# Gated attention and two expert layers on one core: the experts' first product by a Strassen scheme, seven block products for eight

## The chip, the cores and the metric

The kernel runs on one core of a Trainium2 chip. The metric is the device time of one execution in microseconds; of the kernel before there are three timed runs and one profiled execution.

## What is computed

A gated linear attention, then a bilinear layer, then a layer of four experts. The part that the change touches is the last (x is the output of the bilinear layer, 3072 tokens of 384):

```python
def _moe2_ref(x, domain_probs, w1, w2) -> np.ndarray:
    N, D = x.shape
    E = w1.shape[0]
    p = domain_probs / (domain_probs.sum(-1, keepdims=True) + 1e-09)
    out = np.zeros((N, D), dtype=np.float32)
    for e in range(E):
        h = np.maximum(x @ w1[e], 0.0)
        out += p[:, e:e + 1] * (h @ w2[e])
    return out.astype(np.float32)
```

There are 4 experts, w1[e] is 384 x 1024, w2[e] is 1024 x 384.

## The kernel before

The kernel issues each engine's instructions by hand, in program order, with semaphores between engines. Everything is held transposed: features lie on the 128 partitions, tokens along the columns.

Every product is made of split values: a number is its rounded part (`hi`) plus a rest (`lo`), and a block product is three matmuls, hi by hi, hi by lo, lo by hi (`TERMS`). The hi parts come from ScalarE copies, the lo parts from a difference on VectorE or GpSimd.

*The stage before.* Attention and bilinear layer run together over 4 batches of 768 tokens. A step of the bilinear layer (`up1`, `down1`, `bilinear`) is 27 matmuls of 384 columns: 18 for the two products a and b into banks 0 and 1, and 9 into banks 2 to 4. ScalarE copies a, VectorE multiplies (L838), ScalarE rounds (L607), GpSimd takes the difference g_lo (L528). Each half batch ends with x1, whose hi and lo parts are stored to DRAM by the sync engine (SP). In the last half batch ScalarE and GpSimd also split the first expert's weights (`pieces_high` L578, `pieces_low` L517), 1024 columns a step.

*The experts' stage.* The loops are: expert, pair of token tiles ("round", 512 tokens each tile), tile, and column block f of the 8 blocks of 128 in the 1024. A step (`step2`) is one tile and one f: 9 up matmuls (L1221, three input blocks of 128 by three terms) into bank 0 or 1 by turns, for the step after next, and 9 down matmuls (L1339) into three banks that gather over the 8 f. In `step2` a down matmul and an up matmul follow each other one by one. When a bank is full, VectorE applies relu and gate (L1036), ScalarE rounds to h_hi (L731), VectorE takes h_lo (L1040). For expert 0, ScalarE reads the bank itself (L617) and the gate comes in the sum. After 8 f VectorE adds three banks to `total` in SBUF (L1026, L1028). x1 is loaded from DRAM again for each expert, 24 times hi and lo; the weights of the next expert are loaded in one piece while the present one runs.

At the border of the stages the first up product is issued ahead of the last `down1` (in `bilinear`, where `last_batch and beside and s == STEPS1 - 1`), the second behind it.

## Time and profile before

| | |
|---|---|
| three timed runs, median | 1203.96 us (1203.85 to 1204.05) |
| the profiled execution | 1203.85 us |
| its span, first to last instruction | 1202.1 us |
| granted TensorE clock, mean | 1.000 |
| busy: TensorE / VectorE / ScalarE / GpSimd | 1196.4 / 549.1 / 287.1 / 161.2 us |
| experts' stage | from 413.3 us to the end |

The span is what lies between the first and the last instruction; the execution takes 1.75 us more. "PE" is TensorE's matmuls, "PEld" its weight loads, which run beside the matmuls; DVE is VectorE, ACT ScalarE, POOL GpSimd, and a name with q is that engine's sequencer. A matmul's own duration in the trace reaches past the start of the next, so their pace is read from the starts.

### The profile page before, as it was taken

The page shows a single profiled execution, that of the slowest core. Times are in us where ns is not written, and L with a number is a line of the kernel's source. Part 1 is how long each engine was busy: PE and PEld are TensorE (multiplying, and loading weights), DVE is VectorE, ACT ScalarE, POOL GpSimd, SP SyncE. Part 2 cuts the span into 40 slices and gives each one's busy share as a digit, 9 for nine tenths or more (in the row PEclk, how much of TensorE's full clock was granted, in tenths as well). Part 3 has the DMA queues.
Part 4 walks back from the last instruction along what each step waited for, and adds up shares of the span by engine and source line. Part 5 has one row for each costly group of instructions (what it writes and reads, how often), then busy time and mean ns, then how long its engine had stood idle before and what let it go on. Part 6 is the DMA issues. An engine that isn't in the chain of part 4 may idle for free.

```text
span 1202.1 us, 17638 instructions
## 1 busy us (share of the span) xinstructions
PE 1196.4 (100%) x7164; PEld 1038.4 (86%) x7164; DVE 549.1 (46%) x1008; ACT 287.1 (24%) x527; POOL 161.2 (13%) x147
## 2 busy tenths in 40 slices
PE   9999999999999999999999999999999999999998
PEld 7799999999999988888888888888888888888887
DVE  6997686676751112222234434433344344344333
ACT  3443333332323311111111111112112111111111
POOL 1132222222222500000000000000000000000000
PEclk9999999999999999999999999999999999999999
DMA  9744543543613370011151111115011111222201
GB/s 290 208 125 108 143 128 93 159 126 74 164 48 142 117 299 29 26 51 53 53 210 53 53 52 53 53 53 205 19 39 52 53 53 53 79 79 79 79 1 52
DMA packets 89782, 114.34 MB, mean 95 GB/s; under 512 B 39152, under 2 KB 57968, under 8 KB 88688
## 3 DMA queue, kind: packets, MB, share of 16 engines
q1 hardware_dynamic: 89424, 112.97, 30.0%
q8 instruction: 49, 0.80, 0.3%
q10 hardware_dynamic: 288, 0.39, 0.1%
q14 instruction: 21, 0.17, 0.0%
HBM read 92.59 MB, written 18.40 MB: 92 GB/s over the span
## 4 chain that ended last, share of the span: by engine, by line
PE 98%; DVE 1%; DMA 1%; SPq 0%; ACT 0%; issue 0%; DVEq 0%; ACTq 0%
PE bank L1221 33%; PE bank L1339 22%; PE score_banks L1339 11%; PE bank L1068 9%; PE bank L1070 9%; PE bank L1069 9%; PE bank L1109 2%; PE bank L1290 1%; PE score_banks L1130 1%; PE bank L1119 1%; PE score_banks L1093 1%; DMA wo_sb<-w_out 1%; DVE total L1028 0%; PE bank L1077 0%; DVE w_lo L923 0%; DVE suffix L767 0%
## 5 line engine op out<-in xcount | busy, mean ns | idle before, releaser
L1221 PE MATMUL bank<-x_hi,we_lo 128*128 128x512 f32 x576 | 224.1, 389 | 0.0
L1221 PE MATMUL bank<-x_lo,we_hi 128*128 128x512 f32 x576 | 224.1, 389 | 0.0
L1221 PE MATMUL bank<-x_hi,we_hi 128*128 128x512 f32 x576 | 224.1, 389 | 0.0
L1036 DVE SCALAR_TENSOR_TENSOR h_scaled<-bank,gate_rows 128x512 f32<-128x512 f32 (+1 forms) x145 | 99.5, 687 | 246.4 <-PE bank L1221 246.3
L731 ACT ACTIVATE h_hi<-h_scaled 128x512 fp32r<-128x512 f32 (+1 forms) x145 | 91.1, 629 | 484.6 <-DVE h_scaled L1036 484.6
L1339 PE MATMUL bank<-h_hi,we_hi 128*128 128x512 f32 x384 | 149.4, 389 | 0.0
L1339 PE MATMUL bank<-h_lo,we_hi 128*128 128x512 f32 x384 | 149.4, 389 | 0.0
L1339 PE MATMUL bank<-h_hi,we_lo 128*128 128x512 f32 x384 | 149.4, 389 | 0.0
L1040 DVE TENSOR_TENSOR h_lo<-h_scaled,h_hi 128x512 fp32r<-128x512 f32 (+1 forms) x145 | 99.8, 689 | 100.0 <-ACT h_hi L731 100.0
L517 POOL TENSOR_TENSOR we_lo<-we_raw,we_hi (+1 forms) x48 | 61.0, 1292 | 535.4 <-ACT we_hi L578 535.4
L1068 PE MATMUL bank<-x,wb_hi 128*128 128x384 f32 x384 | 128.6, 335 | 0.0
L1070 PE MATMUL bank<-x,wb_lo 128*128 128x384 f32 x384 | 128.3, 334 | 0.0
L1069 PE MATMUL bank<-x,wb_hi 128*128 128x384 f32 x384 | 128.3, 334 | 0.0
L1221 PEld LDWEIGHTS bank<-x_hi,we_lo 128*128 128x128 f32 x576 | 108.1, 188 | 22.5
L1221 PEld LDWEIGHTS bank<-x_lo,we_hi 128*128 128x128 f32 x576 | 108.1, 188 | 22.5
L1221 PEld LDWEIGHTS bank<-x_hi,we_hi 128*128 128x128 f32 x576 | 108.1, 188 | 22.3
L848 DVE SCALAR_TENSOR_TENSOR h_lo<-bank,h_hi 128x512 fp32r<-128x512 f32 x48 | 33.2, 691 | 143.9 <-ACT h_hi L617 143.7
L528 POOL TENSOR_TENSOR g_lo<-g_sb,g_hi 128x384 fp32r<-128x384 f32 x64 | 66.3, 1036 | 221.2 <-ACT g_hi L607 221.2
L838 DVE TENSOR_TENSOR g_sb<-a_sb,bank 128x384 f32<-128x384 f32 x64 | 35.3, 552 | 110.8 <-PE bank L1070 110.8
L1339 PEld LDWEIGHTS bank<-h_hi,we_hi 128*128 128x128 f32 x384 | 72.0, 188 | 15.2 <-DVE h_lo L1040 0.2
L1339 PEld LDWEIGHTS bank<-h_lo,we_hi 128*128 128x128 f32 x384 | 72.0, 188 | 14.9
L1339 PEld LDWEIGHTS bank<-h_hi,we_lo 128*128 128x128 f32 x384 | 72.0, 188 | 14.9
(103 smaller groups left out, 1654.5 us busy)
## 6 DMA issues: line engine op xcount, KB each, us to landing
x_hi<-x_hi_spill SPq DMA_DIRECT2D x24, 768.0 KB, 5.0
x_lo<-x_lo_spill SPq DMA_DIRECT2D x24, 768.0 KB, 6.5
we_raw<-wset SPq DMA_DIRECT2D x4, 3072.0 KB, 10.5
inputs<-akq SPq DMA_DIRECT2D x24, 448.0 KB, 5.1
values<-v_rows SPq DMA_DIRECT2D x24, 256.0 KB, 3.8
gate_rows<-gate_spill SPq DMA_DIRECT2D x4, 1536.0 KB, 13.7
inputs<-akq SPq DMA_DIRECT2D x24, 224.0 KB, 3.3
x_hi_spill<-x_hi_out SPq DMA_DIRECT2D x8, 576.0 KB, 4.2
```

Source lines behind the costliest of these rows:

```text
L517: pool.tensor_tensor(set_lo(n)[:, at], set_raw(n)[:, at], set_hi(n)[:, at], ALU.subtract).then_inc(piece_lo, 1)
L528: pool.tensor_tensor(g_lo[:, s % 2, :], g_sb[:, s % 2, :], g_hi[:, s % 2, :], ALU.subtract).then_inc(g_lo_ready, 1)
L731: act.activation(h_hi[:, s % 2, at], h_scaled[:, s % 2, at], ACT.Copy).then_inc(h_hi_ready, 1)
L838: dve.tensor_tensor(g_sb[:, s % 2, :], a_sb[:, s % 2, :], bank[1][:, 0:TILE1], ALU.mult).then_inc(g_ready, 1)
L848: dve.scalar_tensor_tensor(out=h_lo[:, s % 2, :], in0=bank[s % 2][:, :], scalar=0.0, in1=h_hi[:, s % 2, :], op0=ALU.max, op1=ALU.subtract) ...
L1036: dve.scalar_tensor_tensor(out=h_scaled[:, s % 2, part], in0=bank[s % 2][:, part], scalar=0.0, in1=gate_rows[e % 2][:, at], op0=ALU.max, o ...
L1040: dve.tensor_tensor(h_lo[:, s % 2, part], h_scaled[:, s % 2, part], h_hi[:, s % 2, part], ALU.subtract).then_inc(h_lo_ready, 1)
L1068: pe.matmul(dst, left[0], right[0], start=first, stop=False)
L1069: pe.matmul(dst, left[0], right[1], start=False, stop=False)
L1070: return pe.matmul(dst, left[1], right[0], start=False, stop=last)
L1221: mm = pe.matmul(bank[s % 2][:, :], (we_hi if term < 2 else we_lo)[e % 2][:, cols], (x1_lo if term == 1 else x1_hi)[u][:, k, :], start=(i ...
L1339: mm = pe.matmul(bank[SUM_BANKS[u][part]][:, :], (we_hi if term < 2 else we_lo)[e % 2][:, cols], (h_lo if term == 1 else h_hi)[:, s % 2, : ...
```

## The change

The second product and the stage before stay as they are in what they compute. In the experts' stage:

- The unit is now a group: a pair of tiles p (3), an expert e (4) and a pair of column blocks g (4), 48 in all, tiles outermost. The up product of a group is a matrix of 2 x 3 weight blocks by 3 x 2 token blocks. Over two of the three input blocks it is made of seven products of sums of blocks (a Strassen scheme in Winograd's form), over the third of four plain ones.
- GpSimd makes four sums of weight blocks for each group (`mix_weights`), VectorE four sums of x blocks for each pair of tiles (`mix_x`); the sums are split into hi and lo like the rest.
- The products go alternately to bank 0 (X1 to X4) and bank 1 (Y1 to Y4), and VectorE adds up the four results h in SBUF (`sum_c11` to `sum_c12`), then relu and gate (`make_h`), ScalarE's h_hi, VectorE's `h_low`.
- The output of a pair of tiles gathers in six banks over all experts and is copied out by ScalarE (`out_copy`), the last time one of six by VectorE; the sums into `total` are gone.
- x1 is stored once, unsplit, and loaded once per pair of tiles; the weights are loaded once per pair of tiles and group, 768 KB each. At the border, X1, Y1, X2, Y2 and X3 of the first group are issued ahead of the last `down1` (`begin_experts`). The x of the first pair is mixed and split during the last half batch of the bilinear layer: `mix_x` in its steps 9 and 10, `x_high` from 9 to 13, `x_low` on VectorE from 11 to 13; the first two groups' weights in steps 8 to 11.

The core of the diff (the blocks B and C are blocks of x, A and REST blocks of w1, S and T sums):

```diff
-WSET = 2 * KT * FF
+PAIR2 = 2 * TILE2
...
+W_BLOCKS = 15
+A11, A12, A22, S4, REST1, REST2 = range(6)
+DOWN1, DOWN2, S1, S2, S3 = 6, 9, 12, 13, 14
+A21 = S4
+X_BLOCKS = 9
+B11, B21, C1, T3, B22, C2, T1, T2, T4 = range(X_BLOCKS)
+B12 = T3
+W_PIECES = [slice(4 * P, 8 * P), slice(8 * P, 12 * P), slice(0, 4 * P), slice(12 * P, 15 * P)]
...
+X_SUMS = [(T1, B12, B11), (T2, B22, T1), (T3, B22, B12), (T4, B21, T2)]
+H_AT = [(0, 0), (1, 1), (1, 0), (0, 1)]
...
+            def load_weights(n):
...
+            sp.wait_ge(y_summed, 2)
+            load_weights(FPAIRS - 1)
+            load_x(1, x_loaded[1])
+            for n in range(1, TILE_PAIRS * GROUPS - FPAIRS + 1):
+                p, step = divmod(n, GROUPS)
+                if step == 0 and p + 1 < TILE_PAIRS:
+                    sp.wait_ge(y_summed, 4 * n)
+                    load_x(p + 1, x_loaded[(p + 1) % 2])
+                if step == 0:
+                    sp.wait_ge(evacuated, 2 * KT * (p - 1) + KT)
+                    store_out(p - 1, 0, 0, KT)
+                sp.wait_ge(h_used, 4 * n)
+                load_weights(n + FPAIRS - 1)
+                if step == 0:
+                    sp.wait_ge(evacuated, 2 * KT * p)
+                    store_out(p - 1, 1, 0, KT)
...
+            def mix_weights(p, e, g):
+                slot, n = g % FPAIRS, group_of(p, e, g)
+                raw = w_raw[slot]
+                pool.wait_ge(w_loaded[slot], 16 * slot_loads(p, e, g))
+                pool.tensor_tensor(raw[:, block_of(S1)], raw[:, block_of(A21)], raw[:, block_of(A22)], ALU.add).then_inc(w_mixed, 1)
+                pool.tensor_tensor(raw[:, block_of(S3)], raw[:, block_of(A11)], raw[:, block_of(A21)], ALU.subtract).then_inc(w_mixed, 1)
+                pool.wait_ge(w_mixed, W_MIXED * n + 2)
+                pool.tensor_tensor(raw[:, block_of(S2)], raw[:, block_of(S1)], raw[:, block_of(A11)], ALU.subtract).then_inc(w_mixed, 1)
+                pool.wait_ge(w_mixed, W_MIXED * n + 3)
+                pool.tensor_tensor(raw[:, block_of(S4)], raw[:, block_of(A12)], raw[:, block_of(S2)], ALU.subtract).then_inc(w_mixed, 1)
...
+            def period(p, e, g, lows=None):
+                mix_weights(p, e, g + 2)
+                weights_low(p, e, g + 2, range(len(W_PIECES)))
+                if lows:
+                    x_low(p + 1, lows)
...
+            def first_copy(n):
+                act.wait_ge(x_summed, 4 * n + 1)
+                act.activation(product1[:, :], bank[0][:, :], ACT.Copy).then_inc(x_copied, 1)
+            def h_high(n, i, after_use=True):
+                act.wait_ge(h_ready, 4 * n + i + 1)
+                if after_use:
+                    act.wait_ge(h_used, 4 * (n - 1) + i + 1)
+                act.activation(h_hi[:, i, :], h[:, i, :], ACT.Copy).then_inc(h_hi_ready, 1)
...
+            def period(p, e, g, first=False, prepare=True, prepared=None, drain=None):
+                n = group_of(p, e, g)
+                if not first:
+                    first_copy(n)
+                    h_high(n, 0)
+                if prepare:
+                    weights_high(p, e, g + 2, [0])
+                if drain is not None:
+                    out_copy(drain, 0, 0)
+                    out_copy(drain, 0, 1)
+                    out_copy(drain, 0, 2)
+                if prepare:
+                    weights_high(p, e, g + 2, [1])
+                if prepared:
+                    x_high(p + 1, prepared)
+                h_high(n, 1, not first)
+                if drain is not None:
+                    out_copy(drain, 1, 0)
+                    out_copy(drain, 1, 1)
+                    out_copy(drain, 1, 2)
+                h_high(n, 2, not first)
+                if prepare:
+                    weights_high(p, e, g + 2, [2, 3])
+                h_high(n, 3, not first)
...
+            def mix_x(p, steps):
+                raw = x_raw[p % 2]
+                for i in steps:
+                    if i == 0:
+                        dve.wait_ge(x_loaded[p % 2], 32 * (p // 2 + 1))
+                    else:
+                        dve.wait_ge(x_mixed, X_MIXED * p + i)
+                    to, left, right = X_SUMS[i]
+                    dve.tensor_tensor(raw[:, x_block(to)], raw[:, x_block(left)], raw[:, x_block(right)], ALU.subtract).then_inc(x_mixed, 1)
...
+            def sum_c11(n):
+                dve.wait_ge(x_copied, n + 1)
+                dve.wait_ge(y_summed, 4 * n + 1)
+                dve.tensor_tensor(h[:, 0, :], bank[1][:, :], product1[:, :], ALU.add).then_inc(y_read, 1)
+            def sum_u2(n):
+                dve.wait_ge(x_summed, 4 * n + 2)
+                dve.tensor_tensor(sum2[:, :], bank[0][:, :], product1[:, :], ALU.add).then_inc(x_read, 1)
+            def sum_u4(n):
+                dve.wait_ge(x_read, 4 * n + 1)
+                dve.wait_ge(y_summed, 4 * n + 2)
+                dve.tensor_tensor(h[:, 3, :], bank[1][:, :], sum2[:, :], ALU.add).then_inc(y_read, 1)
+            def sum_u3(n):
+                dve.wait_ge(y_read, 4 * n + 2)
+                dve.wait_ge(x_summed, 4 * n + 3)
+                dve.tensor_tensor(h[:, 1, :], bank[0][:, :], h[:, 3, :], ALU.add).then_inc(x_read, 1)
+                dve.tensor_tensor(h[:, 2, :], bank[0][:, :], sum2[:, :], ALU.add).then_inc(x_read, 1)
+            def sum_c22(n):
+                dve.wait_ge(x_read, 4 * n + 2)
+                dve.wait_ge(y_summed, 4 * n + 3)
+                dve.tensor_tensor(h[:, 1, :], bank[1][:, :], h[:, 1, :], ALU.add).then_inc(y_read, 1)
+            def sum_c21(n):
+                dve.wait_ge(x_read, 4 * n + 3)
+                dve.wait_ge(x_summed, 4 * n + 4)
+                dve.tensor_tensor(h[:, 2, :], bank[0][:, :], h[:, 2, :], ALU.add).then_inc(x_read, 1)
+            def sum_c12(n):
+                dve.wait_ge(y_summed, 4 * n + 4)
+                dve.tensor_tensor(h[:, 3, :], bank[1][:, :], h[:, 3, :], ALU.add).then_inc(y_read, 1)
...
+            def make_h(p, e, n, i):
+                if i == 2:
+                    dve.wait_ge(x_read, 4 * n + 4)
+                else:
+                    dve.wait_ge(y_read, 4 * n + {0: 1, 1: 3, 3: 4}[i])
+                dve.scalar_tensor_tensor(out=h[:, i, :], in0=h[:, i, :], scalar=0.0, in1=gate_row(p, e, H_AT[i][1]),
+                                         op0=ALU.max, op1=ALU.mult).then_inc(h_ready, 1)
...
+            def h_low(n, i):
+                dve.wait_ge(h_hi_ready, 4 * n + i + 1)
+                dve.tensor_tensor(h_lo[:, i, :], h[:, i, :], h_hi[:, i, :], ALU.subtract).then_inc(h_lo_ready, 1)
+            def period(p, e, g, first=False, mixes=None):
+                n = group_of(p, e, g)
+                if not first:
+                    sum_c11(n)
+                    make_h(p, e, n, 0)
+                    sum_u2(n)
+                    sum_u4(n)
+                h_low(n, 0)
+                if mixes:
+                    mix_x(p + 1, mixes[:2])
+                sum_u3(n)
+                sum_c22(n)
+                make_h(p, e, n, 1)
+                sum_c21(n)
+                make_h(p, e, n, 2)
+                h_low(n, 1)
+                sum_c12(n)
+                make_h(p, e, n, 3)
+                h_low(n, 2)
+                h_low(n, 3)
+                if mixes:
+                    mix_x(p + 1, mixes[2:])
...
-            def scaled_low(e, m, s):
-                n = e * ROUNDS + m
-                dve.wait_ge(gate_rows_loaded[e % 2], 16 * (e // 2 + 1))
-                dve.wait_ge(up_done, STEPS2 * n + s + 1)
-                for part in h_parts(e, m, s):
-                    at = bass.ds((2 * m + s // FT) * TILE2 + part.start, part.stop - part.start)
-                    dve.scalar_tensor_tensor(out=h_scaled[:, s % 2, part], in0=bank[s % 2][:, part], scalar=0.0, in1=gate_rows[e % 2][:, at],
-                                             op0=ALU.max, op1=ALU.mult).then_inc(h_scaled_ready, 1)
...
+            def products(dst, done, slot, buffer, blocks, down=None, start=0, count=0):
+                for i, (w, x) in enumerate(blocks):
+                    left = (w_hi[slot][:, block_of(w)], w_lo[slot][:, block_of(w)])
+                    right = (x_hi[buffer][:, x_block(x)], x_lo[buffer][:, x_block(x)])
+                    for term in range(TERMS):
+                        mm = pe.matmul(dst, left[term // 2], right[term % 2], start=i == 0 and term == 0,
+                                       stop=i == len(blocks) - 1 and term == TERMS - 1)
+                        if i == len(blocks) - 1 and term == TERMS - 1:
+                            mm.then_inc(done, 1)
+                        at = TERMS * i + term
+                        if at < count:
+                            down(start + at, 1)
+                if count > TERMS * len(blocks):
+                    down(start + TERMS * len(blocks), count - TERMS * len(blocks))
+            def up_x1(n, g, p, *beside):
+                pe.wait_ge(w_lo_ready, len(W_PIECES) * (n + 1))
+                products(bank[0][:, :], x_summed, g, p % 2, [(A11, B11)], *beside)
+            def up_y1(n, g, p, *beside):
+                products(bank[1][:, :], y_summed, g, p % 2, [(A12, B21), (REST1, C1)], *beside)
+            def up_x2(n, g, p, *beside):
+                pe.wait_ge(x_copied, n + 1)
+                products(bank[0][:, :], x_summed, g, p % 2, [(S2, T2)], *beside)
+            def up_y2(n, g, p, *beside):
+                pe.wait_ge(y_read, 4 * n + 1)
+                products(bank[1][:, :], y_summed, g, p % 2, [(S1, T1)], *beside)
+            def up_x3(n, g, p, *beside):
+                pe.wait_ge(x_read, 4 * n + 1)
+                products(bank[0][:, :], x_summed, g, p % 2, [(S3, T3)], *beside)
+            def up_y3(n, g, p, *beside):
+                pe.wait_ge(y_read, 4 * n + 2)
+                products(bank[1][:, :], y_summed, g, p % 2, [(REST2, C2)], *beside)
+            def up_x4(n, g, p, *beside):
+                pe.wait_ge(x_read, 4 * n + 3)
+                products(bank[0][:, :], x_summed, g, p % 2, [(A22, T4), (REST2, C1)], *beside)
+            def up_y4(n, g, p, *beside):
+                pe.wait_ge(y_read, 4 * n + 3)
+                products(bank[1][:, :], y_summed, g, p % 2, [(S4, B22), (REST1, C2)], *beside)
...
-            def step2(e, m, s, ahead):
-                pe.wait_ge(h_lo_ready, STEPS2 * (e * ROUNDS + m) + s + len(h_parts(e, m, s)))
-                if ahead:
-                    up2_waits(*ahead)
-                for i in range(KT * TERMS):
-                    down2_product(e, m, s, i)
-                    if ahead:
-                        up2_product(ahead[0], ahead[2], i)
...
+                def down(start, count):
+                    for i in range(start, start + count):
+                        if i < 3 * KT * TERMS:
+                            down_product(n - 1, (g - 1) % FPAIRS, KT * TERMS + i, begins=before, ends=ends)
+                        else:
+                            down_product(n, g, i - 3 * KT * TERMS, begins=begins)
+                if not first:
+                    pe.wait_ge(x_read, 4 * n)
+                    if at_start and g == 0:
+                        pe.wait_ge(x_lo_ready, X_BLOCKS * (p + 1))
+                    up_x1(n, g, p, down, 0, 3)
+                    pe.wait_ge(y_read, 4 * n)
+                    up_y1(n, g, p, down, 3, 7)
+                    up_x2(n, g, p, down, 10, 3)
+                    up_y2(n, g, p, down, 13, 4)
+                    up_x3(n, g, p, down, 17, 3)
+                    up_y3(n, g, p, down, 20, 4)
+                    up_x4(n, g, p, down, 24, 6)
+                    up_y4(n, g, p, down, 30, 6)
...
```

## Rows read from the trace of the kernel before

**Rows 1.** The page, busy time, share of the span and instructions of each engine.

```profile
PE 1196.4 (100%) x7164; PEld 1038.4 (86%) x7164; DVE 549.1 (46%) x1008; ACT 287.1 (24%) x527; POOL 161.2 (13%) x147
```

**Rows 2.** A stretch: length; busy PE, PEld, DVE, ACT, POOL (instructions); clock, DMA, GB/s.

```profile
700.00:800.00 100.00, 100.00 (x443) 82.81 (x442) 39.29 (x58) 18.50 (x31) 9.24 (x8) 1.00 0.14 48
```

**Rows 3.** Timeline near 803: start, duration, engine, line, operation [idle before, releaser].

```profile
802.42 0.39 PE L1339 MATMUL bank<-h_hi,we_lo 128*128 128x512 f32 x1
...
802.65 0.39 PE L1221 MATMUL bank<-x_hi,we_lo 128*128 128x512 f32 x1
...
803.15 0.69 DVE L1036 SCALAR_TENSOR_TENSOR h_scaled<-bank,gate_rows 128x512 f32<-128x512 f32 x1 [2.00 <-PE bank L1221]
...
803.87 0.63 ACT L731 ACTIVATE h_hi<-h_scaled 128x512 fp32r<-128x512 f32 x1 [3.45 <-DVE h_scaled L1036]
```

**Rows 4.** The page's groups: operation xcount, busy us, mean ns, idle before.

```profile
L1221 PE MATMUL bank<-x_hi,we_hi 128*128 128x512 f32 x576 | 224.1, 389 | 0.0
```

**Rows 5.** The waits: who waited for whom, us in total, times, longest.

```profile
PEld score_banks L1339 <- DVEq L1057: 0.4, 1, 0.4
```

**Rows 6.** Single lines: duration ns min/median/max, first and last start.

```profile
L1040 DVE TENSOR_TENSOR h_lo<-h_scaled,h_hi x145: 418/692/695, 612.8 to 1196.1; 128x512 fp32r<-128x512 f32 x143, 128x256 fp32r<-128x256 f32 x2
...
L617 ACT ACTIVATE h_hi<-bank x48: 598/598/600, 415.6 to 607.2; 128x512 fp32r<-128x512 f32 x48
...
L578 ACT ACTIVATE we_hi<-we_raw x48: 613/617/632, 385.0 to 992.6; 128x512 fp32r<-128x512 f32 x24, - x24
```

**Rows 7.** Single lines of GpSimd, and its timeline at 390.8.

```profile
L517 POOL TENSOR_TENSOR we_lo<-we_raw,we_hi x48: 1286/1292/1297, 386.1 to 994.1; - x36, 128x512 fp32r<-128x512 f32 x12
...
L528 POOL TENSOR_TENSOR g_lo<-g_sb,g_hi x64: 997/1017/1446, 60.0 to 413.2; 128x384 fp32r<-128x384 f32 x64
...
390.80 2.54 POOL L517 TENSOR_TENSOR we_lo<-we_raw,we_hi 128x512 fp32r<-128x512 f32 x2
```

**Rows 8.** Timeline of the end of the experts' stage.

```profile
1195.74 0.76 DVE L1040 TENSOR_TENSOR h_lo<-h_scaled,h_hi 128x256 fp32r<-128x256 f32 x2 [0.16 <-ACT h_hi L731]
...
1196.55 0.19 PEld L1339 LDWEIGHTS bank<-h_hi,we_hi 128*128 128x128 f32 x1 [0.21 <-DVE h_lo L1040]
1196.60 0.45 PE L1339 MATMUL bank<-h_hi,we_hi 128*128 128x512 f32 x1
...
1197.62 1.98 DVE L1028 TENSOR_TENSOR total<-bank,total 128x512 f32<-128x512 f32 x3 [1.12 <-PE bank L1339]
```

**Rows 9.** The page's DMA issues: count, KB each, median us from issue to landing.

```profile
x_hi<-x_hi_spill SPq DMA_DIRECT2D x24, 768.0 KB, 5.0
x_lo<-x_lo_spill SPq DMA_DIRECT2D x24, 768.0 KB, 6.5
we_raw<-wset SPq DMA_DIRECT2D x4, 3072.0 KB, 10.5
```

**Rows 10.** VectorE lines (ns min/median/max), and timelines of VectorE and GpSimd near 84.

```profile
L854 DVE TENSOR_TENSOR wb_lo<-wb_raw,wb_hi x12: 676/682/1509, 47.5 to 85.0; 128x512 fp32r<-128x512 f32 x12
...
L838 DVE TENSOR_TENSOR g_sb<-a_sb,bank x64: 542/553/555, 58.8 to 412.0; 128x384 f32<-128x384 f32 x64
...
83.84 2.71 DVE L854 TENSOR_TENSOR wb_lo<-wb_raw,wb_hi 128x512 fp32r<-128x512 f32 x3
...
84.56 1.45 POOL L528 TENSOR_TENSOR g_lo<-g_sb,g_hi 128x384 fp32r<-128x384 f32 x1 [2.84 <-ACT g_hi L607]
```

**Rows 11.** Timeline of TensorE at the border of the stages.

```profile
413.33 0.39 PE L1221 MATMUL bank<-x_hi,we_hi 128*128 128x512 f32 x1
...
415.18 0.39 PE L1221 MATMUL bank<-x_hi,we_lo 128*128 128x512 f32 x1
```

**Rows 12.** Timelines of SP, GpSimd and VectorE in the last half batch.

```profile
367.22 0.58 SPq L369 DMA_DIRECT2D we_raw<-wset  x1
...
385.15 1.02 POOL L528 TENSOR_TENSOR g_lo<-g_sb,g_hi 128x384 fp32r<-128x384 f32 x1 [4.02 <-ACT g_hi L607]
...
388.64 0.56 DVE L838 TENSOR_TENSOR g_sb<-a_sb,bank 128x384 f32<-128x384 f32 x1 [3.87 <-PE bank L1070]
```

More of the change, by code:

```diff
@@ new lines, in _ @@
+            for p in range(TILE_PAIRS):
+                last = p == TILE_PAIRS - 1
+                if p >= 1:
+                    dve.wait_ge(first_rows_loaded[p % 2], 16 * (p // 2 + 1))
+                for g in range(FPAIRS):
+                    period(p, 0, g, first=p == 0 and g == 0, mixes=range(X_MIXED) if g == 1 and not last else None)
+                dve.wait_ge(gate_rows_loaded[p % 2], 48 * (p // 2 + 1))
+                with dve.Fori(1, EXPERTS) as e:
+                    for g in range(FPAIRS):
+                        period(p, e, g)
```

548 lines of the change are left out of this document (312 added, 236 removed).

## The prediction

> **What bounds the kernel now.** I read the page's busy times first: TensorE is busy 100% of the span, VectorE 46%, ScalarE 24%, GpSimd 13% [rows 1]. A busy TensorE is not yet TensorE at its pace, so next come a stretch of the experts' stage and the timeline inside it: 443 matmuls begin in 100 us at a granted clock of 1.00 [rows 2], one every 0.2267 us, and up (L1221) and down (L1339) already take turns one by one [rows 3]. The 3456 matmuls of 512 columns (three groups of 576 at L1221 [rows 4], and by its loops 4 x 6 x 8 x 9 = 1728 at L1339 too) make 783.4 us of 1202.1. The list of waits has TensorE waiting only 0.4 us at the stage's start [rows 5] and 0.2 near its end [rows 8]; all long waits there are of the others for TensorE. So the stage costs matmuls times pace, and VectorE's few microseconds of work per step sit in its shadow.
>
> **Matmuls removed.** A group is one pair of token tiles, one expert, two of the eight column blocks: 3 x 4 x 4 = 48 groups. Before, its first product takes 2 x 2 x 3 block products of 3 terms, 36 matmuls. After, seven combined products replace eight over two of the three input blocks and four plain ones do the third: 11 x 3 = 33. The second product stays at 36. So 69 for 72, in all 144 fewer: 144 x 0.2267 = 32.6 us, on the path, since nothing else bounds. A page speaks of this pace: the Trainium skill, TensorE: Matmul & The Clock Gate, section Back-to-back issue gap, gives N/2.4 + 2.5 ns, 216 ns at 512 columns, by which 144 matmuls would be worth 31.1 us; the trace shows 227 and decides.
>
> The order "by turns" gives nothing: the turns are there already [rows 3].
>
> **What is added.** A period (one group) is 69 matmuls, 15.64 us. Per period VectorE gets 8 sums out of the banks, 4 gated relus, 4 differences: 16 operations of 0.69 (L1036 [rows 3], L1040 [rows 6]), 11.1 us or 71%. ScalarE gets a bank copy (0.60, L617), four h_hi (0.63, L731 [rows 3]), four pieces of weights (0.62, L578) [rows 6], 5.6 us. GpSimd gets four sums of 128 columns and four differences; from 1.29 at 512 columns and 1.02 at 384 [rows 7] I extrapolate 0.48 at 128 (an estimate), 6.8 us. None fills the period. VectorE sits idle anyway, so this is free unless it delays a bank.
>
> And it can: the first product now has two banks, each of which must be read before the next product but one. The prices for that schedule: last matmul of a bank starts at 802.65, VectorE starts on it at 803.15, 0.50 later; VectorE's start to ScalarE's 0.72 [rows 3]; VectorE's operations with no wait between follow 0.61 to 0.64 apart (three totals in 1.98 [rows 8]); VectorE done to weight load 0.05, and a weight load that comes late still lets its matmul run some 0.11 later (h_lo ends at 1195.74 + 0.76 = 1196.50, load at 1196.55, its matmul reads 0.45 instead of 0.39 [rows 8]).
>
> Count the period's matmuls from 0. X1 owns 0 to 5, Y1 6 to 18, X2 19 to 24, Y2 25 to 31, X3 32 to 37, Y3 38 to 44, X4 45 to 56, Y4 57 to 68; the last up matmul of each is 4, 16, 23, 29, 36, 42, 55, 67. By 0.2267 each:
> - C11 after Y1: 4.13 to 4.82. Y2 needs it at 5.67. Gated relu 0: to 5.6.
> - U2 after X2: 5.71 to 6.40. X3 needs it at 7.25.
> - U4 after Y2: 7.07 to 7.76. Y3 needs it at 8.61. Then difference 0: 7.68 to 8.37.
> - U3 (two operations) after X3: 8.66 to 9.96. X4's first weight load wants to go at 9.97; the release reaches it at 10.01, and 0.11 later is 10.12, against a matmul due at 10.20. Margin 0.08.
> - C22, relu 1, C21, relu 2, difference 1 (15.0, due 15.6), C12 16.4 (due 17.0), relu 3, differences 2 and 3, to 18.5; the next period needs VectorE at 19.77.
>
> So one gate is tight, X4 behind U3, and the others have 0.6 or more. ScalarE does its work between these points; weights for group n+3 are asked for at 11.8 of period n and land some 5 us later (768 KB as x_hi, 5.0 [rows 9]), two periods ahead of use.
>
> **The tight gate under contention.** Operations of VectorE that read two tensors in SBUF wait for a GpSimd operation: the difference L854 takes 1509 ns at most for a median of 682, a triple of it at 83.84 took 2.71 with a 1.45 g_lo of GpSimd from 84.56 within it, and g_lo itself (1446 at most for 1017 [rows 7]) was held. An operation that reads a bank and one tensor (L838) never left 542 to 555 [rows 10]. That is what the Trainium skill states in SBUF — State Buffer, section Who interferes with whom: two SBUF inputs contend with a GpSimd instruction that reads SBUF, and the lock holds for the whole instruction; the trace agrees. Here the relus, the differences and the mixing of x are exposed, the eight sums are not. ScalarE's piece 0 ends near 6.8, GpSimd's difference of it runs from 6.9 to 8.2, and difference 0 of VectorE arrives at 7.68: it ends at 8.2 plus 0.56 (83.84 + 2.71 = 86.55 against 84.56 + 1.45 = 86.01 [rows 10]), near 8.8, and U3 starts at 8.7 in place of 8.66. With the margin of 0.08 the loss is 0 to 0.2 per period. I take 0.1 for 45 periods: 4.5 us. Bounds: 0, and 0.7 where GpSimd's difference starts just ahead of VectorE's (29 us).
>
> **The mixing of x** for the next pair lies in VectorE's second period of pairs 0 and 1. Two dependent operations, 0.72 each, stand between difference 0 and U3, from 8.4 to 9.8: U3 and X4 come 1.1 late, twice. For pair 1 of tiles the data are late besides: the x1 store of 576 KB, at about 421, lands 4 to 5 later (768 KB take 5.0), then 768 KB of weights and 1536 KB of x are issued from 425.5. 3072 KB take 10.5 and the second 768 KB of an x pair 6.5 [rows 9], so I put the landing near 434.8, and the mixing could start at 434.1: 0.9 more. Together 3.1 us (2.2 to 6). GpSimd's and ScalarE's extra work on x in six periods adds collisions with relu 0 and difference 0; 0.3 each, 1.8 us (0 to 6).
>
> **The seam.** Before, 9 up matmuls run ahead of the last down1 from 413.33 [rows 11], and 0.4 is lost behind it [rows 5]. After, 18 run there (X1 to X3 with no down between). Y2 then follows Y1 by X2's three matmuls only: C11 takes 0.50 + 0.69 + 0.16 = 1.35 from Y1's last start against 0.91 of matmuls, 0.4 lost. Behind down1, X4 has only Y3's three matmuls ahead of it, and VectorE comes to U3 near 419.1, after C11, U2, relu 0, U4 and difference 0, and leaves it at 420.4 against 420.1: with the release another 0.5. Sum 0.9. The stage before is left as it is: x0_lo, the gate and g_lo keep their places; x splits go into VectorE's idle 4.1 of each 4.7 us step [rows 12], GpSimd's mixing delays g_lo by up to 0.8 where it has 2.5 (it ends at 386.2, and the down that reads it follows the product that frees g_sb at 388.64 [rows 12]). Set and x are asked for at 367 to 370, as the set is now (367.22 [rows 12]), and are used at 385 (L578 [rows 6]) and 389. If x came after 391, each microsecond would count. The x1 spill is stored once instead of twice, hidden before and after.
>
> **The end.** 27 downs without ups; their second nine wait for difference 2, about 0.2. After the last matmul a 0.60 copy replaces a 0.69 sum ahead of the store: 0.1 less. Net 0.1.
>
> **Sum.** The profiled execution: 1203.85, span 1202.1 (1.75 around it), median 1203.96. 1203.85 - 32.6 + 4.5 + 3.1 + 1.8 + 0.9 + 0.1 = 1181.7; I predict 1181.5.
>
> **Rivals.**
> - *Clean.* No steady loss at X4, collisions fall elsewhere: 1203.85 - 32.6 + 4.1 = 1175.4, 1172 to 1177.
> - *The collision costs more.* Relu 0 is itself held by GpSimd's mixing, and shifts piece 0 to 7.3, so that difference 0 ends at 9.1: 0.3 to 0.45 per period, 14 to 20 us: 1192 to 1198; at the bound of 0.7, 1206. For it: nothing locks the two engines' phases. Against: when GpSimd starts later than 7.68, VectorE goes first and loses nothing.
> - *Slower.* GpSimd's differences 0 and 1 follow 1.25 apart (2.54 for two [rows 7]). If the second takes the port ahead of the waiting VectorE, difference 0 ends at 10.1, U3 comes 1.35 late: 45 x 1.3 = 58, less 32.6: 1235. It turns slower from 0.55 per period on. By the skill's same section, issue order decides who blocks; at 84.56 to 86.55 GpSimd waited for one VectorE operation and went ahead of the next, so the two alternate, and this speaks against it.
> - *It doesn't do what it says*: the 33 matmuls pace slower than the 36 did. In a run of nine ups from 413.33 to 415.18 the pace is 0.231 [rows 11], 2% slower than by turns, but such runs are rare after as before; all 3312 at that pace would cost 14 us, 1196.
>
> **How the numbers follow.** Forecast (1177 to 1190) 0.55; clean 0.12; costlier collision (1190 to 1206) 0.19, of it 0.13 below 1201.5; slower by the port 0.12; no gain for another reason 0.02. The range for 8 in 10 takes in forecast, clean and the costlier collision up to 1203: 1172 to 1203. About 0.2% is what this measurement can tell (2.4 us): faster, below 1201.5, 0.80; same 0.06; slower 0.14.
>
> **What would show it.** TensorE: 69 matmuls per period at 0.2267, 3312 of 512 columns; in the list of waits an idle time of TensorE ahead of X4, released by VectorE's second U3 sum, near 0.1 per period and over 1 us twice. VectorE's differences and relus with maxima above 0.69, the sums without. GpSimd's differences stretched. Wrong would be: idle time ahead of another product than X4, an idle that is mostly ScalarE's or a weight's, or a pace other than 0.2267.

## The result and the profile after

The changed kernel takes 1186.53 us (median of four runs, 1185.09 to 1188.06) against 1204.01 (1203.85 to 1204.77): 0.9854 of the time before, 95% interval 0.9837 to 0.9871. It is faster by 1.5%, which is clear of the interval, and 5.0 us above the number predicted, inside its range. The profiled execution is the fastest of the four, 1185.09 us, span 1183.4, granted clock 0.998. The working below is against it and against the 1203.85 of before; the other three took 1.4 to 3.0 us longer and have no trace, so what they lost besides is not shown.

The page, busy time of each engine, answers to [rows 1]:

```profile
PE 1170.3 (99%) x7020; PEld 1011.6 (85%) x7020; DVE 889.0 (75%) x1364; ACT 405.0 (34%) x762; POOL 540.8 (46%) x501
```

TensorE has 144 instructions fewer. VectorE works 889 us instead of 549, and TensorE is still the engine that fills the span. A steady stretch, columns as in [rows 2], has as many matmuls as before:

```profile
820.00:920.00 100.00, 100.00 (x443) 82.76 (x442) 78.51 (x104) 31.04 (x56) 53.56 (x49) 1.00 0.17 53
```

The list of waits says where TensorE stood (who waited for whom: us in total, times, longest). In the experts' stage L1053 is the second U3 sum, L1037 the sum C11, L1041 the sum U2:

```profile
PEld bank L1456 <- DVE h L1053: 7.3, 6, 2.7
...
PEld bank L1456 <- DVE h L1037: 2.0, 6, 0.6
PEld bank L1456 <- DVE sum L1041: 1.8, 6, 0.5
```

The first row is X4's: six waits, not 45. One is in the seam, four are in the periods in which the next pair's x is prepared, and only one (931) is in the other periods. The forecast steady loss isn't there, and a few places lose more than forecast. One of the tighter steady periods, VectorE, GpSimd and TensorE near 803 (start, duration):

```profile
802.77 0.69 DVE L1046 TENSOR_TENSOR h<-bank,sum 128x512 f32<-128x512 f32 x1 [0.74 <-PE bank L1456]
803.38 1.13 DVE L1264 TENSOR_TENSOR h_lo<-h,h_hi 128x512 fp32r<-128x512 f32 x1
804.43 0.68 DVE L1052 TENSOR_TENSOR h<-bank,h 128x512 f32<-128x512 f32 x1
805.03 0.67 DVE L1053 TENSOR_TENSOR h<-bank,sum 128x512 f32<-128x512 f32 x1
...
802.66 2.99 POOL L593 TENSOR_TENSOR w_lo<-w_raw,w_hi 128x512 fp32r<-128x512 f32 x2 [1.04 <-ACT w_hi L681]
...
805.67 0.39 PE L1621 MATMUL bank<-h_hi,w_lo 128*128 128x512 f32 x1
805.90 0.40 PE L1456 MATMUL bank<-x_hi,w_hi 128*128 128x512 f32 x1
```

The collision is there as described: difference 0 takes 1.13 us beside GpSimd's difference. But U3 ends at 805.70, and X4's first matmul (805.90) follows its predecessor by 0.23, the usual distance. In 39 of the 48 periods difference 0 ends 1.83 to 1.85 us behind the start of GpSimd's first difference, so its length depends on how far ahead GpSimd is. It is 0.91 to 1.03 in most of them, where U3 ends 0.26 to 0.35 ahead of X4's start; 1.12 to 1.13 in six, where that is 0.19 to 0.21; and 1.46 at 928.53, where ScalarE also copies out tiles and GpSimd starts only 0.39 ahead. There X4 waits, and 0.3 us are lost. Where X4 waits, it starts 0.05 after U3's end.

The large losses lie where x is mixed for the next pair (L1012, two dependent operations of VectorE ahead of U3):

```profile
433.49 3.01 POOL L593 TENSOR_TENSOR w_lo<-w_raw,w_hi 128x512 fp32r<-128x512 f32 x2 [0.40 <-ACT w_hi L681]
...
434.10 1.25 DVE L1264 TENSOR_TENSOR h_lo<-h,h_hi 128x512 fp32r<-128x512 f32 x1
435.27 2.51 DVE L1012 TENSOR_TENSOR x_raw<-x_raw 128x512 f32<-128x512 f32 x2
437.69 0.68 DVE L1052 TENSOR_TENSOR h<-bank,h 128x512 f32<-128x512 f32 x1
...
436.39 0.39 PE L1621 MATMUL bank<-h_hi,w_lo 128*128 128x512 f32 x1
439.03 0.50 PE L1456 MATMUL bank<-x_hi,w_hi 128*128 128x512 f32 x1 [2.25 <-DVE h L1053]
```

TensorE's starts are 2.64 apart instead of 0.23, and the late matmul costs 0.11 more: 2.5 us. At 692.18 the same costs 2.3. Behind the first of the two gaps, and not behind the second, the granted clock falls (columns as in [rows 2], then TensorE's timeline):

```profile
440.00:444.00 4.00, 4.00 (x13) 3.10 (x12) 1.14 (x3) 0.63 (x1) 0.00 (x0) 0.57 0.50 151
```

```profile
441.10 0.63 PE L1621 MATMUL score_banks<-h_hi,w_hi 128*128 128x512 f32 x1
441.53 0.63 PE L1456 MATMUL bank<-x_lo,w_hi 128*128 128x512 f32 x1
```

Matmuls start 0.43 apart from 440.3 to 443.7, the lower level of the clock (1.2 GHz of 2.4): eight distances, 1.6 us.

**The balance.** From the first up matmul to the last matmul there were 785.15 us (413.33 [rows 11] to 1198.48), and there are 763.24 (414.31 to 1177.55): 21.9 less, so of 32.6 us of removed matmuls 10.7 are lost again. The first up matmul comes 1.0 later than before, and 5.82 us lie behind the last matmul's start instead of 3.65. So -32.6 + 10.7 + 1.0 + 2.2 = -18.7, and the executions differ by 18.76. Summing every distance between two starts that is over the usual one gives 10.3 of the 10.7.

### The profile page after: what moved, and what is told of

It reads as the page before. It is cut to its first block, busy times and chain, and to the rows that moved or that the text cites. A ratio compares the mean times of both kernels' runs of the same rounds, so it can differ in the third digit from the quotient of the medians.

```text
span 1183.4 us, 18598 instructions
## 1 busy us (share of the span) xinstructions
PE 1170.3 (99%) x7020; PEld 1011.6 (85%) x7020; DVE 889.0 (75%) x1364; ACT 405.0 (34%) x762; POOL 540.8 (46%) x501
## 4 chain that ended last, share of the span: by engine, by line
PE 95%; DVE 3%; POOL 1%; issue 0%; ACT 0%; DVEq 0%; ACTq 0%
PE bank L1456 30%; PE bank L1621 21%; PE score_banks L1621 11%; PE bank L1309 9%; PE bank L1311 8%; PE bank L1310 8%; PE bank L1350 2%; PE bank L1566 1%; PE score_banks L1371 1%; PE bank L1360 1%; PE score_banks L1334 1%; POOL w_lo L593 1%; PE bank L1548 1%; DVE h_lo L1264 1%; POOL g_lo L603 0%
## 5 line engine op out<-in xcount | busy, mean ns | idle before, releaser
L593 POOL TENSOR_TENSOR w_lo<-w_raw,w_hi 128x512 fp32r<-128x512 f32 x192 | 274.0, 1448 | 292.3 <-ACT w_hi L681 292.3
L745 ACT ACTIVATE h_hi<-h 128x512 fp32r<-128x512 f32 x192 | 121.5, 633 | 503.6 <-DVE h L1080 503.6
L1456 PE MATMUL bank<-x_hi,w_hi 128*128 128x512 f32 x528 | 207.7, 393 | 5.2 <-DVE h L1053 4.9
L1456 PE MATMUL bank<-x_lo,w_hi 128*128 128x512 f32 x528 | 205.8, 390 | 0.0
L1456 PE MATMUL bank<-x_hi,w_lo 128*128 128x512 f32 x528 | 205.7, 390 | 0.0
L1264 DVE TENSOR_TENSOR h_lo<-h,h_hi 128x512 fp32r<-128x512 f32 x192 | 195.9, 1039 | 0.3
L1621 PE MATMUL bank<-h_hi,w_hi 128*128 128x512 f32 x384 | 149.6, 390 | 0.0
L1621 PE MATMUL bank<-h_hi,w_lo 128*128 128x512 f32 x384 | 149.6, 390 | 0.0
L1621 PE MATMUL bank<-h_lo,w_hi 128*128 128x512 f32 x384 | 149.5, 389 | 0.0
L1080 DVE SCALAR_TENSOR_TENSOR h<-h,gate_rest 128x512 f32<-128x512 f32 x144 | 115.3, 801 | 7.1 <-DVE h L1037 1.5
```

The source lines that it names most:

```text
L593: pool.tensor_tensor(w_lo[slot][:, at], w_raw[slot][:, at], w_hi[slot][:, at], ALU.subtract).then_inc(w_lo_ready, 1)
L745: act.activation(h_hi[:, i, :], h[:, i, :], ACT.Copy).then_inc(h_hi_ready, 1)
L1080: dve.scalar_tensor_tensor(out=h[:, i, :], in0=h[:, i, :], scalar=0.0, in1=gate_row(p, e, H_AT[i][1]), op0=ALU.max, op1=ALU.mult).then_inc ...
L1264: dve.tensor_tensor(h_lo[:, i, :], h[:, i, :], h_hi[:, i, :], ALU.subtract).then_inc(h_lo_ready, 1)
L1456: mm = pe.matmul(dst, left[term // 2], right[term % 2], start=i == 0 and term == 0, stop=i == len(blocks) - 1 and term == TERMS - 1)
L1621: mm = pe.matmul(bank[SUM_BANKS[t][m]][:, :], (w_hi if term < 2 else w_lo)[g][:, w], (h_lo if term == 1 else h_hi)[:, quarter, :], start=b ...
```

## The experiments

**1. The mixing behind hidden block 1.** Does X4 wait for the mixing, or would it wait anyway?

```diff
-                if mixes:
-                    mix_x(p + 1, mixes[:2])
                 sum_u3(n)
                 sum_c22(n)
                 make_h(p, e, n, 1)
+                if mixes:
+                    mix_x(p + 1, mixes[:2])
```

> Edit: in VectorE's period the first two sums of x blocks (mix_x) stand behind C22 and relu 1 instead of ahead of U3; the last two stay at the period's end. Theory (the gate of U3): the changed kernel's two idle gaps of TensorE ahead of X4, 2.64 us between starts at 436.4 and 2.38 at 692.2, come from these two operations (2.51 us both times) and vanish; with the first goes the stretch at half clock from 440.3 to 443.7 (1.8 us). In all 6.0 to 6.7 us less than the changed kernel: about 1179 to 1180, and the spread between its runs (1185 to 1188) shrinks with the clock at 1.000. Rival (late data): x has landed only at 434.6 for pair 1, and what waits on it shifts with it: the first gap stays above 1 us. Rival (next gate): the two sums now delay C21 or difference 1 and the gap comes back ahead of X1 or of a down, less than 3 us gained.

Measured: 1179.48 us (1178.96 to 1180.24), 0.9795 of before (0.9779 to 0.9812), 7.1 below the change. TensorE at the former gap, and VectorE's mixing:

```profile
436.16 0.39 PE L1621 MATMUL bank<-h_hi,w_lo 128*128 128x512 f32 x1
436.39 0.44 PE L1456 MATMUL bank<-x_hi,w_hi 128*128 128x512 f32 x1
...
437.54 1.41 DVE L1012 TENSOR_TENSOR x_raw<-x_raw 128x512 f32<-128x512 f32 x2
```

Both gaps are gone, no other of their size took their place (the largest is 0.70 between starts, and Y2 and X3 now wait 0.2 each near 448 and 450), the two operations take 1.41 instead of 2.51, and the clock stays at 1.00. The losses of the stage fall from 10.3 to 4.3 us. So X4 waited for the mixing ahead of U3, and the rivals of late data and of a next gate are refuted at this size. The move also took the mixing away from GpSimd's differences; experiment 2 parts the two.

**2. ScalarE rounds x ahead of the weights in these periods.** The mixing keeps its place, but GpSimd has nothing to do beside it, since its differences wait for ScalarE. This parts the cost of the place from that of the port, by which I mean what VectorE's operations with two operands in SBUF and GpSimd's wait for each other on.

```diff
+                if prepared:
+                    x_high(p + 1, prepared)
                 if prepare:
                     weights_high(p, e, g + 2, [0])
...
                     weights_high(p, e, g + 2, [1])
-                if prepared:
-                    x_high(p + 1, prepared)
```

> Edit: in the periods in which ScalarE splits x, it does so ahead of the two pieces of weights instead of behind them, so that GpSimd's two differences of weights start some 2.7 us later and no longer lie beside VectorE's difference 0 and its two sums of x blocks, which stay ahead of U3. Theory (shared port): the two sums take 1.4 us together instead of 2.5, difference 0 takes 0.7 instead of 1.0 to 1.25, and each of the two gaps ahead of X4 shrinks from 2.3 us of loss to 1.1 to 1.3; at that length the stretch at half clock may vanish too. Gain 2.2 to 4 us against the changed kernel. Rival (the sums are slow by themselves, two dependent operations in place in the same tile): they keep 2.5 us and the gaps keep their length.

One run: 1180.95 us.

```profile
434.12 0.68 DVE L1264 TENSOR_TENSOR h_lo<-h,h_hi 128x512 fp32r<-128x512 f32 x1
434.76 1.42 DVE L1012 TENSOR_TENSOR x_raw<-x_raw 128x512 f32<-128x512 f32 x2
...
434.76 2.71 ACT L691 ACTIVATE x_hi<-x_raw 128x512 fp32r<-128x512 f32 x5 [1.83 <-DMA x_raw<-x_spill]
```

The difference takes 0.68 instead of 1.25 and the mixing 1.42 instead of 2.51. The distances at X4 fall from 2.64 and 2.38 to 1.02 and 0.97, a loss of 0.9 each with the late matmul behind, near the 1.1 that the prediction had for the place. The rest, some 1.5 each, was GpSimd at the port; that the sums are slow by themselves is refuted. The gain is 4.1 us against the profiled run of the change, at the top of the 2.2 to 4 expected: 3.0 from the gaps and 1.6 from the clock, which does not fall here, less 0.5 that small gaps elsewhere and a later start of the stage take (the losses of the stage are 6.0).

**3. The end in smaller stores.** The last pair's first tile leaves in three transfers as its columns are ready.

```diff
-            sp.wait_ge(evacuated, 2 * KT * last + KT)
-            store_out(last, 0, 0, KT)
+            for i in range(KT):
+                sp.wait_ge(evacuated, 2 * KT * last + i + 1)
+                store_out(last, 0, i, 1)
...
```

> Edit: the last pair's first tile is stored in three transfers of 256 KB, each as soon as its copy is done, instead of one of 768 KB behind the third copy. In the changed kernel the last matmul starts 5.85 us before the end of the span, in the kernel before 3.65. Theory (the large store stands ahead of the last small ones): the first two thirds leave 1.4 and 0.7 us earlier, the last store lands in about 2 to 3 us instead of 4.1, and the end comes 1 to 2 us sooner: about 1185 median. Rival (the sync engine's issuing is the bound: four issues from 1176.6 to 1180.1, six now): no gain or 0.5 us lost.

Measured: 1184.29 us (1182.73 to 1185.04), 0.9835 (0.9819 to 0.9852), by medians 2.2 below the change. From the last matmul to the end of the span it takes 4.45 us instead of 5.82, so 1.4 is the end's. The profiled executions differ by 2.4, since the clock didn't fall in this one. The DMA view of the last microseconds, from 1194 before and from 1176 in the change (busy tenths in slices of a fortieth of 9 and 8 us, and what was moved):

```profile
DMA  0000000000000000000000099999999920000000
...
DMA packets 432, 0.79 MB, mean 87 GB/s; under 512 B 48, under 2 KB 48, under 8 KB 432
```

```profile
DMA  0000000008999999999999999999970000000000
...
DMA packets 833, 1.58 MB, mean 198 GB/s; under 512 B 64, under 2 KB 64, under 8 KB 832
```

Before, 0.79 MB leave at the end; after it is 1.58 MB, since both tiles of a pair gather in banks until the last expert, and the DMA engines are full from 1177.8 on, for over 4 us. Before the change they were full for 2 us, so the longer end is those bytes. In the change they start 0.2 us behind the last matmul; in this experiment, 1.5 us ahead of it.

**4. X1's three matmuls twice (72 per period).** What is a matmul worth in the new order? This gives back the number of matmuls that the change removed, and the output stays the same.

```diff
+                for term in range(TERMS):
+                    pe.matmul(bank[0][:, :], (w_hi if term < 2 else w_lo)[g][:, block_of(A11)], (x_lo if term == 1 else x_hi)[p % 2][:, x_block(B11)],
+                              start=term == 0, stop=term == TERMS - 1)
                 products(bank[0][:, :], x_summed, g, p % 2, [(A11, B11)], *beside)
```

> Edit: X1's three matmuls are done twice (the first time overwritten by the second), so that a period has 72 matmuls as before the change, with all else as in the changed kernel. Theory (matmuls times pace): 144 more at 0.2267 cost 32.6 us, and since the gaps of the changed kernel hang on the spacing from X3 and Y2 to X4, which stays, they remain: 1217 to 1220. That also says that the change without its saving costs 13 to 15 us. Rival (slack absorbs): the three matmuls at the head of the period give VectorE time, part of the losses goes, and the cost is 25 to 29 us. Rival (pace): the added run of one kind slows the pace to 0.231, 34 us or more.

One run: 1215.18 us, 30.1 above the profiled run of the change and below the 1217 to 1220 expected. TensorE's losses are 8.1 instead of 10.3: the small gaps are fewer, as all other engines have 0.7 us more per period. 30.1 and 2.2 make 32.3, against 144 x 0.2267 = 32.6. So a matmul costs its full pace in the new order too, to 0.3 us in 144, and the slack that the expectation named as a rival took a small part of it back.

**5. The four mixings in two periods.** Two of them stand behind hidden block 1 of the second period and two of the third, and ScalarE's and GpSimd's x work is moved to the periods behind them.

```diff
-                if mixes:
-                    mix_x(p + 1, mixes[:2])
                 sum_u3(n)
                 sum_c22(n)
                 make_h(p, e, n, 1)
+                if mixes:
+                    mix_x(p + 1, mixes)
...
-                if mixes:
-                    mix_x(p + 1, mixes[2:])
...
-                    period(p, 0, g, first=p == 0 and g == 0, mixes=range(X_MIXED) if g == 1 and not last else None)
+                    period(p, 0, g, first=p == 0 and g == 0, mixes=range(2 * g - 2, 2 * g) if g in (1, 2) and not last else None)
```

> Edit: the four sums of x blocks are spread over VectorE's second and third period of a pair, two behind relu 1 in each, where the trace of the changed kernel shows VectorE idle for 1.4 us and GpSimd idle too; ScalarE's and GpSimd's splits of the four sums move one period later. Theory (what is left after the first edit is C11 and relu 0 behind the last two sums at a period's end): the idle pairs of TensorE at 447.3 to 453.2 and 699.4 to 705.3 of the kernel with only the first two sums moved (1.3 us each of lost time) vanish: 2 to 2.6 us less than its 1179.5, about 1177. Rival (GpSimd's x splits, not the sums, make these losses by holding difference 0 and relu 0): they stay or move to the period after, within 0.8 us of 1179.5.

Measured: 1180.02 us (1179.04 to 1181.53), 0.9805 (0.9788 to 0.9821), no gain over experiment 1. GpSimd and VectorE:

```profile
460.19 6.41 POOL L642 TENSOR_TENSOR x_lo<-x_raw,x_hi 128x512 fp32r<-128x512 f32 x4
...
465.43 1.72 DVE L1264 TENSOR_TENSOR h_lo<-h,h_hi 128x512 fp32r<-128x512 f32 x1
```

GpSimd now splits x four and five times in a row beside the next difference and relu, and U3 comes late there: two new distances of 0.7 at X4 for each pair, in place of the one that experiment 1 had left. About 1177 had been expected; the rival held: the load on the port is moved, not removed.

**6. Experiment 5 with the end of experiment 3.**

> Edit: the spread sums together with the last pair's first tile stored in three transfers. Theory: the two gains are in different places and add: 1.4 us less than the spread kernel, 1175 to 1176, and 0.976 of the kernel before. Rival: the end is set by issuing, so that less than 0.5 us is added.

Measured: 1178.49 us (1177.59 to 1179.79), by medians 1.5 below experiment 5, though the ranges overlap, and above the 1175 to 1176 expected. From the last matmul to the end of the span it takes 4.38 us, and 5.80 in experiment 5: the end's gain adds up. The two profiled executions don't show it in their sums, 1179.79 against 1179.37, since the first up matmul comes at 415.47 here and at 413.98 there.

**7. One more operation that reads a bank, ahead of U3.** It measures the margin at X4: 0.6 us are added in every period.

```diff
...
+                dve.tensor_tensor(scratch[:, 0:TILE2], bank[0][:, :], h[:, 3, :], ALU.add)
                 dve.tensor_tensor(h[:, 1, :], bank[0][:, :], h[:, 3, :], ALU.add).then_inc(x_read, 1)
```

> Edit: in every period one more VectorE operation (bank 0 plus a tile, into a scratch tile, 0.6 us) stands ahead of the two of U3. It reads one tensor in SBUF only. Theory (X4's gate has a margin of about 0 in every period): each of 48 periods loses 0.55 to 0.62 us: 26 to 30 us more than the changed kernel, 1212 to 1217, that is slower than the kernel before. Rival (the gate has slack that the trace hides, 0.3 or more): less than 15 us more.

One run: 1208.26 us, slower than before the change. That is 23.2 above the profiled run of the change, where 26 to 30 had been expected and less than 15 by the rival.

```profile
799.73 0.69 DVE L1052 TENSOR_TENSOR bilinear_weights_rest<-bank,h 128x512 f32<-128x512 f32 x1
...
801.67 0.50 PE L1457 MATMUL bank<-x_hi,w_hi 128*128 128x512 f32 x1 [0.17 <-DVE h L1054]
```

A period like this one loses 0.44 (0.33 idle by the starts, and 0.11 for the late matmul). 0.60 were added, so 0.16 us of margin were left, counted as in the prediction, with the 0.11 in it. The gate is tight as forecast, and the steady loss isn't there by that little.

**8. One more operation with two operands in SBUF, ahead of U3.**

```diff
...
+                dve.tensor_tensor(scratch[:, 0:TILE2], h[:, 0, :], h_hi[:, 0, :], ALU.subtract)
                 sum_u3(n)
```

> Edit: the same place, but the added operation reads two tensors in SBUF (the difference of h and h_hi, into scratch). Theory (the port alternates): GpSimd's second difference of weights waits for the port while VectorE's difference 0 holds it, so the added operation stands behind it and takes 1.2 to 1.9 us instead of 0.6: 1.2 to 1.8 lost per period, 55 to 85 us more than the changed kernel, 1240 to 1270. Rival (VectorE keeps the port for its next operation): as the edit with a bank, 26 to 30 us more. Rival (GpSimd always first): difference 0 itself lengthens too.

One run: 1248.53 us, inside the 1240 to 1270 expected.

```profile
798.40 3.00 POOL L593 TENSOR_TENSOR w_lo<-w_raw,w_hi 128x512 fp32r<-128x512 f32 x2 [0.95 <-ACT w_hi L681]
...
799.33 0.92 DVE L1264 TENSOR_TENSOR h_lo<-h,h_hi 128x512 fp32r<-128x512 f32 x1
800.17 1.77 DVE L1277 TENSOR_TENSOR bilinear_weights_rest<-h,h_hi 128x512 f32<-128x512 f32 x1
```

The two ends fit taking turns at the port. GpSimd's first difference alone takes 1.29 [rows 7] and ends at 799.69; VectorE's difference ends 0.56 later (799.33 + 0.92 = 800.25). GpSimd's second one runs to 801.40, and the extra operation ends 0.54 behind that (801.94), though it had been waiting since 800.17. An extra operation that reads a bank costs 0.60 and this one 1.70.

**9. Experiments 1 and 3 together.**

> The changed kernel with the first two mixes moved behind hidden block 1 (as in e1_mix_moved, whose profiled run had a span of 1177.3 us and a median of 1179.5) and the last pair's first tile stored in three transfers of 256 KB (as in e3_tail, which took 1.4 us from the stretch between the last matmul and the end). Theory (the two gains lie in different stretches and add): 4.4 to 4.6 us after the last matmul, span near 1176, median 1177.7 to 1178.5, so 8.0 to 8.8 below the changed kernel. Rival (the end is set by the landing of the very last store, which the smaller transfers only helped in one run): no gain over e1_mix_moved, 1179.0 to 1180.0.

Measured: 1178.22 us (1176.64 to 1178.67), 0.9778 (0.9762 to 0.9794): 1.3 below experiment 1, with ratios whose intervals overlap. From the last matmul to the end of the span it is 4.41 us, and 5.81 in experiment 1; the profiled spans differ by 0.6 only, since the first up matmul comes at 414.82 here and at 414.04 there, in a stage that neither edit touches.

**10. U3 ahead of difference 0 as well.** X4 waits for U3 alone.

```diff
-                h_low(n, 0)
                 sum_u3(n)
+                h_low(n, 0)
                 sum_c22(n)
```

> e9_moved_tail with one more edit: in every period VectorE sums U3 before it makes the low part of hidden block 0. In the profile of e1_mix_moved TensorE still lost about 4.3 us in the experts' stage, some 1.3 of it near 447 to 453 and as much near 699 to 705, where the difference of block 0 took 1.71 us beside GpSimd and U3 stood behind it. Theory (X4 waits for U3 alone, and the difference has room): U3 ends 0.9 to 1.7 earlier in every period, most of these 2.6 us go, and the rest of the stage keeps the matmuls 0.2267 apart: 1175.3 to 1176.7, so 1.5 to 2.8 below e9_moved_tail. Rival (the low part of block 0, or the hidden blocks behind it, are then late for the second products): small gaps at the second products' weight loads in many of the 48 periods, 0.1 each is 4.8 in all, and the time is equal to or above e9_moved_tail.

Measured: 1176.32 us (1175.85 to 1177.11), 0.9765 (0.9748 to 0.9781), 10.2 below the change. TensorE at X4 of the third period in experiment 9 and here:

```profile
453.30 0.39 PE L1622 MATMUL bank<-h_hi,w_lo 128*128 128x512 f32 x1
454.00 0.50 PE L1457 MATMUL bank<-x_hi,w_hi 128*128 128x512 f32 x1 [0.32 <-DVE h L1054]
```

```profile
453.10 0.40 PE L1622 MATMUL bank<-h_hi,w_lo 128*128 128x512 f32 x1
453.33 0.40 PE L1457 MATMUL bank<-x_hi,w_hi 128*128 128x512 f32 x1
```

The gaps at X4 are gone, 0.6 each at 453 and 705. For the later difference TensorE waits only once in the seam and once in the last group, 0.6 and 0.3, where it waited 0.4 and 0.3 in the change. What is left of losses, 3.5 us, is 0.9 in the seam and waits of Y2 and X3 for C11 and U2 where a relu stood beside GpSimd's x work: of the 2.6 us that I had put down to U3 only 1.2 were. By medians the gain over experiment 9 is 1.9, by the profiled spans 1.3, and the intervals of the two ratios overlap; the vanished gaps show it, the times alone don't.

## Why the prediction held, and where its terms were off

The sum, 1181.7, was right to 3.4 us of the profiled run (4.8 of the median), and partly by luck, since errors cancelled:

| step | forecast | measured |
|---|---|---|
| 144 matmuls | -32.6 | -32.6 (32.3 in experiment 4) |
| X4 behind U3, 45 periods | 4.5 | 0.3 (one period) |
| mixing of x, twice | 3.1 | 4.8 |
| clock behind the first of these gaps | not seen | 1.6 |
| the other x periods | 1.8 | 2.7 |
| seam | 0.9 | 0.9 |
| stage before | 0 | 1.0 |
| end | 0.1 | 2.2 |
| small rest | 0 | 0.3 |
| sum | -22.2 | -18.8 |

- **Matmuls.** Held, pace and worth. The rival of a slower pace is refuted: 443 matmuls in 100 us, as before.
- **The tight gate.** The mechanism was right (difference 0 is held, to 0.91 to 1.03 in most periods and to 1.13 in some, and X4 alone is close), the size was not, and this is the largest miss. By the prediction's own numbers U3 slips from 8.66 to 8.7 and the margin is 0.08, which gives no loss; the 0.1 per period was chosen on top of them from a range of 0 to 0.2, and no row carried it. Experiment 7 measured a margin of 0.16 where difference 0 took 0.92. For this term the rival "clean" was right.
- **The mixing.** Two mistakes of opposite sign. I charged 0.72 for each of two operations, though I had written that the mixing is exposed to the port: beside two of GpSimd's differences they took 2.51, and the difference ahead 1.25 instead of 0.69. Experiment 2 gives the share, 1.5 us of each gap. And I added 0.9 for late data: they landed at 434.57 as forecast (434.8), but VectorE came to the mixing at 435.27, so it waited for nothing. The forecast had VectorE ready for the mixing at 434.1, without the hold on difference 0 that it counts elsewhere (0.56 here) and without the later start of the stage.
- **The clock.** A gap of TensorE was costed at its length. One of two was followed by 3.4 us of half clock, which cost 1.6. No row of before has such a gap in this stage, so the bound of that term should have been open upward.
- **The other x periods.** 1.8 for 2.7, within its bounds of 0 to 6.
- **The seam.** The sum held, in part by luck. Y2's first matmul is late by 0.5, for 0.4 forecast. X4 waits for U3, which ended at 421.17 where I had 420.4 (the stage began 1.0 later), but loses 0.1 for 0.5. And a second product waits for difference 1 (L1264) at 426.50, 0.3, which wasn't forecast.
- **The stage before.** I put the delay of g_lo at up to 0.8 where it had 2.5. GpSimd and TensorE near 403:

```profile
398.77 3.01 POOL L593 TENSOR_TENSOR w_lo<-w_raw,w_hi 128x512 fp32r<-128x512 f32 x2
401.75 1.45 POOL L603 TENSOR_TENSOR g_lo<-g_sb,g_hi 128x384 fp32r<-128x384 f32 x1
...
402.56 0.34 PE L1311 MATMUL bank<-x,wb_lo 128*128 128x384 f32 x1
403.25 0.44 PE L1309 MATMUL bank<-g_hi,wp_hi 128*128 128x384 f32 x1 [0.35 <-POOL g_lo L603]
```

TensorE waits for g_lo and loses 0.6. ScalarE had g_hi ready at 399.44, but g_lo stood behind two differences of weights, which with VectorE's x differences beside them (three took 4.95 from 398.80) took 3.01 instead of 2.54, and took 1.45 itself instead of 1.02. These 0.6 us are in all eleven profiles of kernels with the change. Another 0.3 arose in the first microseconds of the kernel, which the change doesn't touch and which vary: in the other ten profiles they are between 0.04 less and 1.1 more than before, so of the 1.0 only the 0.6 is shown to be the change's.
- **The end.** After X4's the largest miss. I compared a copy with a sum and didn't ask how many bytes leave behind them: twice as many as before. In [rows 8] nothing shows it; what does is the loop order in the code, by which the second tile's sum of before was the only store left.
- **Rivals.** "Slower by the port" is refuted as a steady cost: GpSimd's second difference doesn't pass the waiting VectorE, they take turns. Experiment 8 shows what it costs when VectorE has two such operations in a row, +62 us. The mixing has that form, twice.

The Trainium skill, SBUF — State Buffer, section Who interferes with whom, says that a VectorE instruction with two inputs in SBUF contends with a GpSimd instruction that reads SBUF, and that one with at most one such input doesn't: experiments 7 and 8 agree, 0.60 against 1.70 us for the same columns, and the bank-reading sums stay at 0.695 at most in the whole stage.

Open stays why the clock fell where it did (below), and 0.3 us in the first microseconds and 0.3 in the small rest.

## What to carry to other kernels

When work is cut from the bound engine and given to an idle one, look for the one buffer that is freed last in each period, count its margin from the trace, and keep every operation that this buffer doesn't need behind it: moving two mixings and one difference behind U3 brought 9 of the 10 us that the best version gained with the new end. Price an operation with two SBUF operands by what GpSimd does at that moment, and two in a row by a full GpSimd operation more. At the end of a kernel, count the bytes that leave behind the last matmul.

## What the hardware showed beyond that

- **Half clock after a short gap, not always.** TensorE's idle time, and the granted clock around its end: idle 2.25 us, fell for 3.4 us (the change, first pair); 1.99, did not (second pair); 2.21 and 1.97, did not (experiment 3); 1.98, did not, and 1.98, fell (experiment 4, its two pairs); 3.10 and 2.59, did not (experiment 7); 3.09, fell for 6.8 us, from 0.7 us before the next matmul on, and 2.59, did not (experiment 8). So a gap of 2 us may cost nothing more or another 1.6 us, and the length of the gap alone doesn't decide. The experiments without such gaps have a mean clock of 1.000 in their profiles.
- **The port is handed over after each operation**, so the wait of one VectorE operation is at most one of GpSimd's, 1.29 us here (no operation of VectorE with two operands in SBUF takes over 1.79 in the experts' stage of the change, for 0.69 alone), and a further one in a row can pay again.
- **GpSimd pays as well:** its differences of 512 columns, 1.29 alone, reach 1.82, and its busy time in the best version is 19 us below the change's with the same 501 instructions.
